# Attention and a gated MLP on one core: a third product with v in fp32r halves, and three steps of the splitting moved to GpSimd

## What is computed

```python
q_rot, k_rot = rotate(q), rotate(k)          # x1*cos - x2*sin, x1*sin + x2*cos
scores = scale * q_rot @ k_rot.T
attn = exp(scores - max(scores)); attn = attn / (sum(attn) + 1e-9)
x = attn @ v                                 # to (2304, 512)
h = x @ w_in                                 # (2304, 1024)
e = exp(h - max(h)); solu = h * e / (sum(e) + 1e-9)
ln = (solu - mean) / sqrt(var + 1e-6) * g_ln
out = ln @ w_out                             # (2304, 512)
```

## Time and profile before

| | us |
|---|---|
| median of 3 runs | 485.28 |
| lowest and highest | 484.88, 485.31 |
| the profiled execution | 485.69 |
| its span on the core | 483.6 |
| TensorE busy | 474.4 (98%) |
| VectorE busy | 375.4 (78%) |
| ScalarE busy | 263.7 (55%) |
| GpSimd busy | 221.7 (46%) |

### The profile page before, as it was taken

One profiled execution on the slowest core, in us unless ns is written; L12 is line 12 of the kernel. 1 busy time (PEld: TensorE's weight loads), 2 busy tenths in 40 slices (PEclk: granted clock), 3 DMA queues, 4 the chain that ended last, 5 costly groups with the idle time before them and its releaser, 6 DMA issues.

```text
span 483.6 us, 7879 instructions
## 1 busy us (share of the span) xinstructions
PE 474.4 (98%) x2555; PEld 402.4 (83%) x2555; DVE 375.4 (78%) x592; ACT 263.7 (55%) x398; POOL 221.7 (46%) x283
## 2 busy tenths in 40 slices
PE   7899999999999999999999999999999999999997
PEld 6678888988898888889888878888888888888885
DVE  6867887888879788878886366999997899888731
ACT  4667787777787778877786343032224222322221
POOL 6778565757575756666571012343343121122110
PEclk9999999999999999999999999999999999999999
DMA  8403455545454555445434203233333223322232
GB/s 289 186 18 76 139 159 112 175 136 169 101 152 150 150 143 148 148 115 179 123 80 100 58 15 58 32 82 67 86 69 80 47 50 69 84 54 62 60 78 86
DMA packets 101008, 50.60 MB, mean 105 GB/s; under 512 B 90280, under 2 KB 90280, under 8 KB 99048
## 3 DMA queue, kind: packets, MB, share of 16 engines
q1 hardware_dynamic: 100152, 50.00, 38.6%
q10 hardware_dynamic: 816, 0.10, 0.1%
HBM read 33.33 MB, written 4.79 MB: 79 GB/s over the span
## 4 chain that ended last, share of the span: by engine, by line
PE 94%; DVE 2%; DMA 1%; ACT 1%; issue 0%; SPq 0%; DVEq 0%; ACTq 0%
PE ps L1145 20%; PE ps L1159 20%; PE ps L1131 19%; PE ps L1082 18%; PE ps L1053 8%; PE ps L1111 5%; PE ps L1097 4%; DMA X<-x_in 1%; DVE nm L822 1%; DVE QK L797 1%; ACT p_main L633 0%; DVE X L763 0%; ACT QK L580 0%; DVE w_lo L846 0%; DVE X L768 0%
## 5 line engine op out<-in xcount | busy, mean ns | idle before, releaser
L822 DVE TENSOR_REDUCE nm<-ps 128x1 fp32r<-128x576 f32 x144 | 108.0, 755 | 34.0 <-PE ps L1053 31.8
L1131 PE MATMUL ps<-p_main,V 128*128 128x288 f32 x400 | 113.6, 406 | 0.0
L1145 PE MATMUL ps<-w_hi,KB 128*128 128x512 f32 x288 | 91.4, 390 | 0.0
L1159 PE MATMUL ps<-w_hi,QK 128*128 128x512 f32 x288 | 91.0, 389 | 0.0
L1082 PE MATMUL ps<-QK 128*128 128x288 f32 x320 | 89.0, 359 | 0.8 <-ACT p_main L633 0.5
L633 ACT ACTIVATE p_main<-ps 128x576 f32<-128x576 f32 x100 | 65.1, 651 | 36.4 <-PE ps L1082 34.7
L409 POOL TENSOR_TENSOR X<-X,rope 128x1152 f32<-128x1152 f32 x26 | 68.6, 2662 | 32.9 <-DVE KB L807 32.7
L1131 PEld LDWEIGHTS ps<-p_main,V 128*128 128x128 f32 x400 | 70.2, 189 | 10.7 <-ACT p_main L633 0.2
L1082 PEld LDWEIGHTS ps<-QK 128*128 128x128 f32 x320 | 55.3, 189 | 18.4 <-issue 5.7
L1082 PE MATMUL ps<-KB 128*128 128x288 f32 x320 | 67.8, 293 | 0.0
L654 ACT ACTIVATE X<-ps,neg_max 128x1024 f32<-128x1024 f32 x18 | 20.1, 1118 | 84.5 <-DVE neg_max L867 84.5
(11 more groups left out here) (114 smaller groups left out, 726.9 us busy)
## 6 DMA issues: line engine op xcount, KB each, us to landing
X<-x_in SPq DMA_DIRECT2D x13, 1152.0 KB, 5.2
V<-oe SPq DMA_DIRECT2D x213, 32.0 KB, 1.9
V<-v_in SPq DMA_DIRECT2D x32, 160.0 KB, 2.7
out<-X SPq DMA_DIRECT2D x18, 256.0 KB, 2.3
w_raw<-w_in SPq DMA_DIRECT2D x16, 256.0 KB, 3.0
xT<-x_in SPq DMA_DIRECT2D x2, 1152.0 KB, 10.8
xT<-oe SPq DMA_DIRECT2D x16, 144.0 KB, 2.4
inv<-inv_rows SPq DMA_DIRECT2D x16, 144.0 KB, 3.0
```

Of the source, the lines that this page charges most:

```text
L822: nc.vector.tensor_reduce(nm[g][:, at:at + 1], src[:, :, 0:HALF], AX_XY, ALU.max, negate=True)\
L1131: ins = nc.tensor.matmul(o_ps[a][:, half, 0:HALF], v, p[:, half * HALF:(half + 1) * HALF], start=(k == 0), stop=(k == 9))
L1145: ins = nc.tensor.matmul(h_ps[t % 3][:, half, :], left[a][:, c, :], right[:, col:col + 512], start=(c == 0 and k == 0), stop=(c == KC - 1 ...
L1159: ins = nc.tensor.matmul(y_ps[a], left[a][:, c * P:(c + 1) * P], right[:, col:col + 512], start=(i == 0), stop=(i == DOWNS - 1))
```

## The change

- Product k = 1 is made of halves too, in pairs 2 to 14; k = 3 is in pairs 1 to 14 as before, k = 8 in pairs 2 to 14. So there is a third pair of v_hi, v_lo, a third `halve_v` on GpSimd, and a third exp into PSUM, copy to p_hi and low_p.
- ScalarE's `take_o(n - 1, 1)` stands ahead of exp of step 1, since exp now writes into the banks that it reads.
- low_queries of B move from VectorE to GpSimd, ahead of the rotation (for pairs from 3 on).
- The high keys of both heads move from ScalarE to GpSimd (`high_keys`), so `set_high` writes the queries alone. low_keys on VectorE and copy_keys on ScalarE wait for `high_k_done`.
- GpSimd's order for pair n becomes: low_queries(n + 1, B), rotate(n + 2), high_keys(n + 2, A), second_queries, a wait for VectorE's low_keys(n + 2, A), divide(n - 2), set_tails, high_keys(n + 2, B), and three times halve_v.
- VectorE's w_low(0) moves from step 6 to step 7 of pair 1.

```diff
-HALVED = (3, 8)
+HALVED = (1, 3, 8)
...
         def halved(n, k):
-            return k in HALVED and 1 <= n < PAIRS - 1
+            return k in HALVED and (1 if k == HALVED[1] else 2) <= n < PAIRS - 1
...
             def wait_x(m):
...
                 if m >= 5:
                     sp.wait_ge(second_done, m - 4)
+                    for a in range(2):
+                        sp.wait_ge(high_k_done[a], m - 4)
...
+            def high_keys(m, a):
+                at = COLS[a]
+                pool.wait_ge(score_ready, STEPS * (m - 2) + (STEPS if a else BOTH + 1))
+                nc.gpsimd.tensor_copy(QK[m % 2][own(a), 1, at:at + S], x_of(m)[own(a), 3, :]).then_inc(high_k_done[a], 1)
+                pool.wait_ge(high_k_done[a], m - 2)
...
-            halve_v(1, 0)
-            halve_v(1, 1)
+            halve_v(1, HALVED[1])
             for n in range(1, PAIRS):
+                if n == 1:
+                    pool.wait_ge(low_q_done[1], 3)
+                elif n + 1 < PAIRS:
+                    pool.wait_ge(low_k_done[1], n + 2)
+                    pool.wait_ge(hi_done[1], high(n + 1, 1))
+                    pool.wait_ge(low_q_done[1], n + 1)
+                    low_queries(n + 1, 1)
+                    pool.wait_ge(low_q_done[1], n + 2)
                 if n + 2 < PAIRS:
-                    pool.wait_ge(low_q_done[1], n + 2)
...
                     rotate(n + 2)
                 if n + 2 < PAIRS:
                     pool.wait_ge(rot_done, n + 3)
+                    high_keys(n + 2, 0)
                     second_queries(n + 2)
-                    set_tails(n + 2)
-                if halved(n + 1, HALVED[0]):
-                    halve_v(n + 1, 0)
+                    pool.wait_ge(low_k_done[0], n + 3)
                 if n >= 2:
                     divide(n - 2)
-                if halved(n + 1, HALVED[1]):
-                    halve_v(n + 1, 1)
+                if n + 2 < PAIRS:
+                    set_tails(n + 2)
+                    high_keys(n + 2, 1)
+                for k in HALVED:
+                    if halved(n + 1, k):
+                        halve_v(n + 1, k)
...
             def set_high(m, a):
...
+                if m >= 3:
+                    nc.scalar.activation(QK[c][own(a), 0, at:at + S], x_of(m)[own(a), 1, :], ACT.Copy)\
+                      .then_inc(hi_done[a], 1)
+                    return
...
             def exp(n, s):
...
                     act.wait_ge(o_taken, 2 * n + a)
+                    if s == HALVED[1] and n >= 2:
+                        act.wait_ge(pv_done, PVS * n + HALVED[0] + 1)
...
                 for s in range(STEPS):
+                    if s == 1 and n >= 2:
+                        take_o(n - 1, 1)
                     exp(n, s)
...
-                        if s == 1:
-                            take_o(n - 1, 1)
+                        if s == 1 and n == 1:
+                            take_o(0, 1)
...
             def low_keys(m, a):
...
+                elif m >= 3:
+                    dve.wait_ge(high_k_done[a], m - 2)
...
                     if s == 0:
                         low_keys(n + 1, 1)
-                    if s == 1:
-                        low_queries(n + 1, 1)
+                    if s == 1 and halved(n, HALVED[0]):
+                        low_p(n, HALVED[0])
+                    if n == 1 and s == 1:
+                        low_queries(2, 1)
                     if s == 4 and n >= 2:
                         w_low(n - 1)
-                    if s == 3 and halved(n, HALVED[0]):
-                        low_p(n, 0)
-                    if s == 7 and halved(n, HALVED[1]):
-                        low_p(n, 1)
+                    if s == 3 and halved(n, HALVED[1]):
+                        low_p(n, HALVED[1])
+                    if n == 1 and s == 7:
+                        w_low(0)
+                    if s == 7 and halved(n, HALVED[2]):
+                        low_p(n, HALVED[2])
...
             def row_scores(m, i):
...
                     if m >= 3:
                         pe.wait_ge(second_done, m - 2)
+                        pe.wait_ge(high_k_done[0], m - 2)
```

More of the change, by code:

```diff
@@ L89, in attention_then_mlp @@
         p_lo = sb("p_lo", [P, S], F32R)
-        v_hi = [sb(f"v_hi_{h}", [P, P], F32R) for h in "ab"]
-        v_lo = [sb(f"v_lo_{h}", [P, P], F32R) for h in "ab"]
+        v_hi = [sb(f"v_hi{i}", [P, P], F32R) for i in range(len(HALVED))]
+        v_lo = [sb(f"v_lo{i}", [P, P], F32R) for i in range(len(HALVED))]
         oe = [sb(f"oe{c}", [P, 2, S]) for c in range(2)]
@@ L104, in attention_then_mlp @@
         p_lo_done = sem("p_lo_done")
-        v_hi_done = [sem(f"v_hi_{h}_done") for h in "ab"]
-        v_lo_done = [sem(f"v_lo_{h}_done") for h in "ab"]
+        v_hi_done = [sem(f"v_hi{i}_done") for i in range(len(HALVED))]
+        v_lo_done = [sem(f"v_lo{i}_done") for i in range(len(HALVED))]
         second_done = sem("second_done")
+        high_k_done = [sem(f"high_k_{h}_done") for h in "ab"]
         x_loaded = [sem(f"x_loaded{c}") for c in range(2)]
@@ L217, in halved, with halves, head @@
         def halved(n, k):
-            return k in HALVED and 1 <= n < PAIRS - 1
-        def halves(n, a):
-            return 2 * (n - 1) + a + 1
+            return k in HALVED and (1 if k == HALVED[1] else 2) <= n < PAIRS - 1
+        def halves(n, k):
+            i = HALVED.index(k)
+            return 1 if n == 1 else 3 * (n - 2) + i + 2
+        def head(k):
+            return k // 5
         def high(m, a):
@@ L494, in _ @@
                 nc.gpsimd.memset(V[c][:, 1, :, 0:D], 1.0).then_inc(v_const, 1)
[L495 to L498, removed]
+            for i, k in enumerate(HALVED):
+                nc.gpsimd.memset(v_hi[i][:, other(head(k))].bitcast(F32), 1.0).then_inc(v_const, 1)
+                nc.gpsimd.memset(v_lo[i][:, other(head(k))].bitcast(F32), 0.0).then_inc(v_const, 1)
+            pool.wait_ge(v_const, 10)
             nc.gpsimd.memset(expo[:, :], -0.5).then_inc(const_done, 1)
@@ L804, in low_queries @@
                     dve.wait_ge(hi_done[a], 2)
+                if m >= 3:
+                    dve.wait_ge(hi_done[a], high(m, a))
                 if m == 2 + (1 - a):
@@ L830, in row_max, with low_p @@
                     nc.vector.transpose(nm_row[g][:, :], nm[g][:, :].bitcast(F32)).then_inc(turned[g], 1)
-            def low_p(n, a):
-                dve.wait_ge(p_hi_done, halves(n, a))
+            def low_p(n, k):
+                a = head(k)
+                dve.wait_ge(p_hi_done, halves(n, k))
                 nc.vector.tensor_tensor(p_lo[:, :].rearrange("p (b c) -> p b c", b=2), o_ps[1 - a][:, :, 0:HALF],
@@ L961, in _ @@
                         invert(n - 1)
-                        if n == 1:
-                            w_low(0)
                     if s == 6 and n + 2 < PAIRS:
@@ L1101, in weigh_tails, with weigh_halves @@
                             ins.then_inc(pv_done, 1)
-            def weigh_halves(n, a):
-                pe.wait_ge(v_lo_done[a], n)
-                pe.wait_ge(p_hi_done, halves(n, a))
-                for i, (v, p) in enumerate(((v_hi[a], p_hi), (v_lo[a], p_hi), (v_hi[a], p_lo))):
-                    if i == 2:
-                        pe.wait_ge(p_lo_done, halves(n, a))
+            def weigh_halves(n, k):
+                i, a = HALVED.index(k), head(k)
+                pe.wait_ge(v_lo_done[i], n if i == 1 else n - 1)
+                pe.wait_ge(p_hi_done, halves(n, k))
+                for part, (v, p) in enumerate(((v_hi[i], p_hi), (v_lo[i], p_hi), (v_hi[i], p_lo))):
+                    if part == 2:
+                        pe.wait_ge(p_lo_done, halves(n, k))
                     for half in range(2):
```

30 lines of the change are left out of this document (18 added, 12 removed).

## The result

The changed kernel takes **500.67 us** (median of 5 runs, 500.46 to 501.12) against 485.28 us (median of 5, 484.88 to 485.66): a ratio of 1.0313, 95% interval 1.0301 to 1.0325. The forecast was 502.7 us, with 489 to 507 around it. The profiled execution took 500.46 us with a span of 498.7 us, 15.1 us more than before, at a granted clock of 0.999 as before.

The account below looks back on a forecast made before the run. TensorE was taken to bound the kernel before, GpSimd's loop at 18.2 us a pair after. 485.7 plus 17.9 for pairs 3 to 13, less 0.5, gave 503.1; against the median 502.7 us, range 489 to 507.

Parts of the forecast that it names:

- The loop: GpSimd's cycle per pair, from VectorE's addition through the rotation to the next addition: 18.2 us, longer than TensorE's 16.29 us.
- The two meetings: GpSimd casts beside VectorE's low_queries of A and low_keys of B: each lengthens GpSimd's cycle by some 0.55 us.
- The hold: The rotation's second half blocks VectorE's w_low until its end, 2.1 us, delaying row maximum and addition: 18.2 instead of 17.1 us.
- The first rival: GpSimd's cycle binds, but w_low slips in or is held shortly: 17.1 us a pair, 490 us; chance 0.20.
- The sum: Pairs 3 to 13 pay 17.9 us in full; pairs 1, 2 and 14 together -0.5 us: 502.7 us in all.
- ScalarE's part: One more pass into p_hi at block 1, take_o ahead of exp of step 1: costs 0 to 0.1 us a pair.
- "tie": At block 1's third pass, ScalarE's queue and TensorE both arrive 3.1 us after the score: 0 to 0.1 us a pair.
- ideal 16.29 us a pair: TensorE's pair time after 0.18 us from halves and 0.10 us of waiting gone, from 16.57: the most the change can give.
- rival "faster": VectorE's and GpSimd's meetings fall where GpSimd waits anyway, its cycle staying under 16.29 us: 481.2 us; chance 0.10.

Follow-up runs that it names:

- keys_b_on_gpsimd: Changed kernel, addition in step 4, w_low in step 5, no wait before division, ScalarE copies moved, high keys of A back on ScalarE, of B on GpSimd: 483.95 us.
- high_keys_alone: Kernel before with only the high keys of both heads on GpSimd, in the change's order; no third product, low_queries of B on VectorE: 483.48 us.
- w_low_one_column: Changed kernel with w_low in its old place but made for one column of 512 in pairs 2 to 13: 494.73 us.
- rotation_writes_only: Changed kernel with GpSimd's rotation of pairs 3 to 15 replaced by memsets of about the same length: 488.66 us.
- no_wait_before_division: Changed kernel without GpSimd's wait for low_keys of head A ahead of the division: 495.03 us.
- moves_alone: Changed kernel without the third product in halves; low queries of B and high keys stay on GpSimd, take_o early: 492.73 us.
- loop_fitted: Changed kernel, addition in step 4, w_low in step 5, no wait before division, two ScalarE copies later, only head A's high keys on GpSimd: 483.85 us.
- the third product alone: Changed kernel with all moves undone: low_queries of B on VectorE, high keys on ScalarE, GpSimd in its old order plus one splitting of v: 497.63 us.

## Why the prediction was right

**The loop** is the term that decided, and it came out step for step. From the end of the addition (173.37): low_keys of head A ends after 2.05 us (forecast 2.08), the division after 3.62 (3.59), the rotation after 15.51 (15.69). The two meetings cost 0.42 us (L446) and 0.59 us (L458), where I had put 0.55 for each. From the rotation's end to the addition's end it is 2.49 us (2.55). That closes at 18.00 us; 18.2 was forecast.

**The hold.** w_low was forecast near 2.8 us and took 2.45: the loop was shorter by 0.2 us, so the rotation reached less far over it. For the row maximum behind it TensorE loses 0.9 us at step 6 (188.99 to 190.16, where 0.27 is usual), and 1.4 was forecast. The rows had only shown holds up to 0.5 us, and between 17.1 and 18.2 I chose by the loop's own lag. In the runs the hold lasts until the end of GpSimd's instruction, be it 1.7 us (w_low) or 1.3 us (one column), and it is absent when GpSimd only writes. The Trainium skill, "SBUF — State Buffer", section "Who interferes with whom", says that a VectorE instruction with two SBUF inputs contends with a GpSimd instruction that reads SBUF, not with one that only writes it, and that whoever issues second is fully blocked. These traces agree with it up to 1.7 us, and the memsets (w_low at 0.75 us) bear out the condition that GpSimd reads. The first rival's 17.1 us was a true length of the loop without the hold (16.97 with memsets, 17.36 with w_low moved), but not what this kernel does.

**The sum.** 11 pairs at 1.43 us are 15.8 and not 17.9: the 0.2 us by which a pair came out shorter, eleven times. Pairs 1, 2 and 14 gave -0.6 (forecast -0.5): pair 1 gained 0.8 us (1 forecast), pair 2 lost only 0.2 us (0.8 forecast), and pair 14 gained 0.05 where 0.28 was forecast.

**ScalarE's part was undersized, and TensorE's side of the "tie" with it**, which the loop hid. I wrote that the product that take_o waits for ends as score 1 starts, and that exp starts 0.9 us after the score's start. ScalarE's timeline of the kernel after:

```profile
178.70 0.67 ACT L624 ACTIVATE QK<-X 64x576 fp32r<-64x576 f32 x1
179.38 0.65 ACT L674 ACTIVATE oe<-ps 128x576 f32<-128x576 f32 x1
180.15 0.64 ACT L660 ACTIVATE ps<-ps 128x576 f32<-128x576 f32 x1
```

The score starts at 178.97, take_o 0.41 us after it, exp at 1.18 us. In this trace two things end just before take_o: ScalarE's own copy (L624, 179.37) and the product with v, which TensorE began at 178.22 and whose record ends at 179.35, after the next product has started. The run keys_b_on_gpsimd tells them apart: there ScalarE is idle for 0.59 us until that product, and take_o still comes 0.42 us after the score (153.67 to 154.09). The third pass comes at 182.31, 3.34 us after the score, where I had 3.1.

TensorE's side was short by as much. I took 0.53 us from a score product to the row-maximum product behind it; after a full-precision product it is 0.74 (156.29 to 157.03), so TensorE by itself comes to the third pass after 3.3 us. What the place costs is therefore seen from the score of step 1 to that of step 3, with one full-precision product and one in halves between them. Two such scores in the kernel before, at a place where nothing waits:

```profile
265.22 0.64 PE L1082 MATMUL ps<-QK 128*128 128x288 f32 x2
...
268.80 0.42 PE L1082 MATMUL ps<-QK 128*128 128x288 f32 x2
```

That is 3.58 us, and in the kernel after it is 182.69 - 178.97 = 3.72. So the place costs TensorE 0.14 us a pair, where I had 0 to 0.1, and of the 0.18 us that the third product gives 0.04 are left. Pair 14, which has a third product and no rotation, gained 0.05 us (the 0.10 us of waiting that I had added there was not lost before either: it took 16.48 us, like the pairs of high_keys_alone). Early pairs say the same: from the product of the tails of pair 2 to that of pair 3, before the loop lags, it is 16.43 us in w_low_one_column, rotation_writes_only and no_wait_before_division, and 16.48 in moves_alone, which has no third product.

The "ideal 16.29 us a pair" was therefore out of reach, and some 16.43 us was the least: the best of the runs with a third product has 16.45 us, the high keys without it 16.48. Had the loop fitted, the forecast for the rival "faster" would have promised twice the gain that there was. The 0.03 us do not show in the whole time, since pair 1 takes 17.71 us in loop_fitted and 17.18 in high_keys_alone. What I did not run is a kernel with the fitted order and without the third product, so that its net value in that order stays open.

**The price by parts.** The hold is 1.03 us of the 1.43 us a pair (memsets). The parts overlap: the third product alone costs 1.01 us a pair, the moves alone 0.71, together 1.43. Both push the same rotation over the same w_low.

## What to carry to other kernels

An engine's idle time is not its room: follow the loop that passes through it once per period, with every wait in it, and compare its length with the period; up to there work is nearly free, and past it every tenth counts in full (0.70 us less on GpSimd took 0.72 us off the pair). Where VectorE and GpSimd share such a loop, keep VectorE operations with two SBUF inputs out of the window of a long GpSimd instruction that reads SBUF, or put them behind the operation that others wait for; look for operations whose duration has grown, since such a hold shows as busy time. And try the parts of a change alone: here one of three was worth -0.35% and the other two cost 3.5%.

## What the runs showed of the hardware

- A VectorE operation with two SBUF inputs, issued during a GpSimd instruction that reads SBUF, did its work at that instruction's end, at either size tried: 128x512 took 2.45 us and not 0.75, 128x1 took 1.37 us and not 0.10. The work begins 0.1 to 0.2 us before the recorded end of GpSimd's instruction.
- The hold goes by the instruction and not by the line of the program: cut into four, GpSimd let w_low in between two quarters and took 6.01 us for what took 5.26.
- GpSimd memsets (128x1152, 1.06 us) did not hold w_low (0.75 us), and a VectorE memset (128x511, 0.48 us) was not held by a GpSimd product.
- The one that comes second pays: with the wait ahead of the division gone, low_keys had the port and the division took 1.80 us and not 1.43.
